# Attention, its first pair of heads, and the transfers around it: one change to a fused attention and two-layer-expert kernel

## The chip, the core and the metric

The kernel runs on one core of a Trainium2 chip. A core has five engines that run side by side and wait for one another through semaphores: TensorE (PE, matrix products and transposes), VectorE (DVE), ScalarE (ACT), GpSimd (POOL) and SyncE (SP), which here only issues transfers. Transfers are carried by 16 DMA engines that all the issuing engines share. SBUF is the memory on the core (128 partitions), PSUM holds what TensorE writes (8 banks of 128 x 512 float32), HBM is the memory outside. The metric is the time of one execution on the device in microseconds (us); of several runs the median counts.

## The reference, cut to what matters

```python
# attention: batch 2, 8 heads, 768 rows, head size 64; 16 heads in all
q_bits = (q @ proj > 0); k_bits = (k @ proj > 0)          # 6 bits each
mask   = bucket(q_bits)[:, None] == bucket(k_bits)[None, :]
scores = where(mask, q @ k.T / 8, -1e9)
attn   = softmax(scores); attn_out = attn @ v
# first expert layer (dense), 1536 tokens x 512, inner size 2048
h = x @ w_in;  g = (a0 + a1 h + a2 h^2 + a3 h^3) / (1 + |b0||h| + |b1| h^2 + 1e-6);  x = g @ w_out
# second layer: each token goes to its best of 8 experts
e = argmax(x @ w_gate);  out = prob[e] * (relu(x @ w1[e]) @ w2[e])
```

Products are made in float32 precision by splitting each operand into a high part and a low part (`hi`, `lo`).

## The kernel before, in words

The program has three stages: attention (to about 306 us of the profile), the dense layer (to about 600 us) and the routed experts.

**Attention** works on heads in pairs, 8 pairs. PE's work is written out by hand in slots, 24 to a pair, 201 in all: even slots make a block of scores (L1195, L1196), three slots in four make a chunk of four transposes of exponentials (L1205), and from slot 9 on each slot makes one value product, `pv` (L1217, L1218), which sums into bank 6. A head's output is finished in two halves of six value products; ACT then copies bank 6 out (`o_evict`, L747), and the next `pv` waits for that copy (`o_out`, L1214). ACT makes the exponentials (L730) and the high parts (L739), DVE the maxima (L940) and the low parts (L960).

The next pair is prepared in the slots of the present one, in ten steps (`step`) that share bank 7: four transposes of q and k, copied to `raw` (L717, L928); POOL splits them into `qk_hi` and `qk_lo` (L571, L573); products with `proj` give `bits` (L720), and two products with `sel` give `mask` (L931, L934). The first pair goes through the same ten steps before slot 0. `raw` and `qk_lo` are the same memory, so ACT's copy for pair p waits until the operands of both heads of pair p-1 have landed (L716).

**SP's queue** is one list, in order: the operands of the two heads of a pair (five transfers each, L453 to L457, waiting for the split), their masks (L464), the loads of q and k (L439) and of v (L444), the output rows (L480, L481), the inverse sums, which go out to HBM (`inverse`, L469) and come back spread over partitions (`rb`, L473), and `routed<-blank` (L514): 21 writes of 128 rows of 2,056 bytes that clear the buffer for the routed tokens. After the last pair SP loads the second quarter of the dense layer's weights (L524, L525), which ACT splits from its step n = 6 on (`w_piece(1, 0)`, L762); ACT works in order, so everything behind that split waits for the load.

Of the kernel before, what the change touches and what calls it, by code (L numbers as in the profile page):

```python
# [15 lines left out]
P = 128  # L16
# [34 lines left out]
C_END = C_TILE + NTAB  # L51


def constants():

    c = np.zeros((P, C_END), np.float32)
# [24 lines left out]
def build(nc, q, k, v, proj, w_in, w_out, a, b, w_gate, w1, w2, consts, out):  # L81
    ctx = ExitStack()
    with ctx:
# [63 lines left out]
        vn = [put(f"vn{i}", [P, NT * D], F32) for i in range(2)]  # L147
        vs = [put(f"vs{i}", [P, NT, 2 * D], F32R) for i in range(2)]
        blank = put("blank", [P, ROW], F32)
        bits = put("bits", [P, HALF], BF16)  # L150
# [78 lines left out]
        s_blank = sem("s_blank")  # L229
# [11 lines left out]
        v_split = sem("v_split")  # L241
        prep_pe = sem("prep_pe")
# [102 lines left out]
        TURN_R_AT = 5  # L345
# [23 lines left out]
        def prep_no(p, k):  # L369

            return 10 * p + k if p < 2 else 20 + 11 * (p - 2) + k + (k >= 4)

        def turn_r_no(p):

            return 20 + 11 * p + 4 if p < NPAIR - 2 else 20 + 11 * (NPAIR - 2) + p - (NPAIR - 2)
# [54 lines left out]
        def _(sp):  # L430
            sp.dma_start(cst[:, 0:P], consts[:, 0:P]).then_inc(s_ident, 16)

            def load_qk(p):

                if p >= 2:
                    sp.wait_ge(prep_pe, prep_no(p - 2, 3) + 1)
# [4 lines left out]
            def load_v(n):  # L441

                wait(sp, v_split, 2 * (n - 1))
                sp.dma_start(vn[n % 2][:, :], v_h[n, :, :]).then_inc(s_v[n % 2], 16)  # L444

            def operand_rows(p):

                sp.wait_ge(qk_split, 4 * (p + 1))
                wait(sp, scores_ready, 12 * (p - 1))
                for o in range(2):  # L450
                    own, other = slice(o * D, (o + 1) * D), slice((1 - o) * D, (2 - o) * D)
                    op, landed = operands[p % 2][o], s_op[p % 2][o]
                    sp.dma_start(op[own, 0:2, :].bitcast(F32), qk_hi[own, 0:1, :].bitcast(F32).broadcast_to([D, 2, S])).then_inc(landed, 16)  # L453
                    sp.dma_start(op[other, 0, :].bitcast(F32), qk_lo[own, 0, :].bitcast(F32)).then_inc(landed, 16)
                    sp.dma_start(op[own, 2, :].bitcast(F32), qk_hi[own, 1, :].bitcast(F32)).then_inc(landed, 16)
                    sp.dma_start(op[other, 2, :].bitcast(F32), qk_hi[own, 1, :].bitcast(F32)).then_inc(landed, 16)
                    sp.dma_start(op[own, 3, :].bitcast(F32), qk_lo[own, 1, :].bitcast(F32)).then_inc(landed, 16)  # L457

            def mask_rows(p):

                sp.wait_ge(prep_out, prep_no(p, 9) + 1)
                for o in range(2):
                    own, other = slice(o * D, (o + 1) * D), slice((1 - o) * D, (2 - o) * D)
                    sp.dma_start(operands[p % 2][o][other, 1:4:2, :].bitcast(F32), mask[own, 0:2, :].bitcast(F32)).then_inc(s_op[p % 2][o], 16)  # L464

            def inverse_rows(p):

                sp.wait_ge(prep_out, turn_r_no(p) + 1)
                sp.dma_start(inverse[p, :, :].rearrange("h (t c) -> (h t) c", c=P), rt[0:2 * NT, :]).then_inc(s_inverse, 16)  # L469
                sp.wait_ge(s_inverse, 16 * (p + 1))  # L470
                wait(sp, x_norm, p)
                for o in range(2):
                    sp.dma_start(rb[o * D:(o + 1) * D, :], inverse[p, o:o + 1, :].broadcast_to([D, S])).then_inc(s_rb, 16)  # L473
# [9 lines left out]
            load_qk(0)  # L483
            sp.dma_start(cst[:, P:C_END], consts[:, P:C_END]).then_inc(s_const, 16)
            sp.dma_start(pr_raw[0:D, :], proj).then_inc(s_proj, 16)
            sp.dma_start(pr_raw[D:P, :], proj).then_inc(s_proj, 16)
            load_qk(1)
            load_v(0)
            load_v(1)
# [918 lines left out]
```

## Time and profile before

| what | us |
|---|---|
| median of 3 runs (lowest, highest) | 931.68 (929.39, 936.72) |
| the profiled execution, its own time | 933.58 |
| its span, first to last instruction | 931.8 |
| attention, first block of scores to the last value product | 33.0 to 305.3 |
| PE busy in the span | 805.1 (86%) |
| mean granted TensorE clock | 0.954 of full speed |

The profile gives for each engine what it did and when, and for each idle time what ended it. A time in a row is counted from the start of the span. A matrix product's own row has its duration as modelled; where PE is idle over a stretch this is seen from the idle time before a row. For transfers a row of SPq is the issue, and the time to landing is given apart.

### The profile page before, as it was taken

To read this page: it belongs to the slowest core of one execution; us is meant where nothing else is said; L and a number is where in the kernel's file an instruction comes from. 1 tells how busy PE (TensorE), PEld (TensorE's weight loads), DVE (VectorE), ACT (ScalarE), POOL (GpSimd) and SP (SyncE) were. 2 spreads that over 40 slices of the span, in tenths; PEclk is the share of its full clock that TensorE was granted. 3 is DMA by queue.
4 is the path that set the end of the run, shared out by engine and by line. 5 is a ranking of instruction groups with operands and counts; after the bars stand their busy time and mean duration, and the time that the engine had idled before them with its cause. 6 is when DMAs were issued, how large, how long until landed. Compare 5 with 4: busy or idle time off the path is not lost.

```text
span 931.8 us, 14695 instructions
## 1 busy us (share of the span) xinstructions
PE 805.1 (86%) x4212; PEld 701.0 (75%) x4212; DVE 666.7 (72%) x1068; ACT 641.4 (69%) x1248; POOL 457.3 (49%) x373
## 2 busy tenths in 40 slices
PE   3599999989988989999999997914999999898984
PEld 2488888878878879999999996903777777686763
DVE  1388787777776678787887886172788886895863
ACT  2377677767778887788787765233888887784871
POOL 3213552453347587476575543054357656553453
PEclk9999999999999999999999998856999999899898
DMA  5797688678671302002000300028531014115550
GB/s 140 153 226 190 155 200 213 164 168 212 142 219 37 124 1 64 28 1 91 1 1 1 152 30 1 1 102 329 189 126 45 30 38 183 59 45 200 217 192 16
DMA packets 59444, 104.52 MB, mean 112 GB/s; under 512 B 30622, under 2 KB 32894, under 8 KB 55296
## 3 DMA queue, kind: packets, MB, share of 16 engines
q1 hardware_dynamic: 53888, 92.04, 34.4%
q10 hardware_dynamic: 3024, 5.53, 2.1%
q0 software_dynamic: 2480, 6.31, 1.8%
q8 instruction: 26, 0.43, 0.2%
q14 instruction: 26, 0.21, 0.1%
HBM read 60.52 MB, written 13.71 MB: 80 GB/s over the span
## 4 chain that ended last, share of the span: by engine, by line
PE 52%; DMA 11%; issue 11%; SPq 7%; ACT 6%; DVE 5%; POOL 5%; ACTq 2%; DVEq 1%; POOLq 0%
PE ps L1252 4%; PE ps L1251 4%; PE ps L1253 4%; PE ps L1267 4%; PE ps L1269 4%; PE ps L1268 4%; DMA out<-yo,gi 4%; DMA operand<-mask 4%; PE ps L1205 4%; PE ps L1369 3%; PE ps L1370 3%; PE ps L1371 3%; PE ps L1195 2%; PE ps L1217 2%; PE ps L1196 2%
## 5 line engine op out<-in xcount | busy, mean ns | idle before, releaser
L960 DVE TENSOR_TENSOR ptl<-ps,pth 128x512 fp32r<-128x512 f32 x144 | 99.7, 692 | 46.6 <-ACT pth L739 43.7
L739 ACT ACTIVATE pth<-ps 128x512 fp32r<-128x512 f32 x144 | 86.1, 598 | 53.3 <-PE ps L1205 52.5
L856 ACT ACTIVATE e1h<-wraw 128x512 fp32r (+1 forms) x160 | 88.0, 619 | 34.2 <-DMA wraw<-in_moe_w 16.4
L940 DVE TENSOR_REDUCE negmax<-ps 128x1 f32<-128x768 f32 x96 | 91.4, 952 | 23.1 <-PE ps L1196 21.7
L631 POOL TENSOR_TENSOR hw<-hw,ha 128x384 f32<-128x384 f32 x64 | 65.6, 1025 | 83.2 <-ACT hw L803 83.2
L856 ACT ACTIVATE e2h<-wraw 128x512 fp32r (+1 forms) x152 | 86.2, 624 | 14.9 <-PE ps L1371 13.0
L730 ACT ACTIVATE pr<-ps,negmax 128x768 f32<-128x768 f32 x96 | 86.5, 901 | 14.1 <-DVE negmax L940 14.1
L1123 DVE TENSOR_TENSOR e1l<-wraw,e1h 128x512 fp32r<-128x512 f32 x120 | 78.8, 719 | 17.5 <-ACT e1h L856 17.3
L1205 PE MATMUL ps<-cst,pr 128*128 128x128 f32 x576 | 89.2, 276 | 1.2 <-ACT pr L730 1.2
L676 POOL TENSOR_TENSOR e2l<-wraw,e2h 128x512 fp32r<-128x512 f32 x38 | 51.3, 1353 | 79.0 <-DVE e2l L1123 53.6
L1251 PE MATMUL ps<-xh,wih 128*128 128x384 f32 x256 | 87.5, 342 | 2.0 <-DVE hp L996 2.0
L1123 DVE TENSOR_TENSOR e2l<-wraw,e2h 128x512 fp32r<-128x512 f32 x114 | 85.7, 817 | 4.1 <-issue 2.7
L1217 PE MATMUL ps<-pth,vs 128*128 128x384 f32 x192 | 77.9, 405 | 12.3 <-issue 6.0
L1252 PE MATMUL ps<-xl,wih 128*128 128x384 f32 x256 | 87.0, 340 | 0.0
L1253 PE MATMUL ps<-xh,wil 128*128 128x384 f32 x256 | 87.0, 340 | 0.0
L1195 PE MATMUL ps<-operand 128*128 128x384 f32 x192 | 70.8, 369 | 13.3 <-DMA operand<-mask 13.3
L1369 PE MATMUL ps<-e2h,hth 128*128 128x512 f32 x152 | 64.6, 425 | 18.4 <-DVE htl L1110 18.4
L426 POOL TENSOR_TENSOR gl<-ha,gh 128x384 fp32r<-128x384 f32 x64 | 65.4, 1022 | 27.9 <-ACT gh L420 27.8
L1267 PE MATMUL ps<-woh,gh 128*128 128x512 f32 x192 | 76.0, 396 | 3.0 <-POOL gl L426 3.0
L1205 PEld LDWEIGHTS ps<-cst,pr 128*128 128x128 f32 x576 | 72.2, 142 | 7.9 <-ACT pr L730 2.3
L1269 PE MATMUL ps<-woh,gl 128*128 128x512 f32 x192 | 75.5, 393 | 0.0
L1268 PE MATMUL ps<-wol,gh 128*128 128x512 f32 x192 | 75.5, 393 | 0.0
(170 smaller groups left out, 2221.1 us busy)
## 6 DMA issues: line engine op xcount, KB each, us to landing
wraw<-in_moe_w SPq DMA_DIRECT2D x32, 1024.0 KB, 8.7
operand<-qk_hi SPq DMA_DIRECT2D x16, 384.0 KB, 4.9
operand<-qk_lo SPq DMA_DIRECT2D x32, 192.0 KB, 4.3
operand<-qk_hi SPq DMA_DIRECT2D x32, 192.0 KB, 4.5
operand<-mask SPq DMA_DIRECT2D x16, 384.0 KB, 6.3
routed<-blank SPq DMA_DIRECT2D x21, 257.0 KB, 4.8
xg<-routed ACTq DMA_DIRECT2D x21, 257.0 KB, 2.7
wi_raw<-in_moe_w_in SPq DMA_DIRECT2D x4, 1024.0 KB, 6.1
```

The lines of the kernel that those rows point to most:

```text
L856: act.activation(E_HI[x][:, k, :], raw_piece(at, x, k), ACT.Copy).then_inc(e_hi[x], 1)
L960: dve.tensor_tensor(ptl[:, at:at + CW], ps[:, 4 + c % 2, :], pth[:, at:at + CW].bitcast(F32), ALU.subtract).then_inc(ptl_done, 1)
L1123: dve.tensor_tensor(E_LO[x][:, k, :], raw_piece(at, x, k), E_HI[x][:, k, :].bitcast(F32), ALU.subtract).then_inc(e_lo_dve[x], 1)
L1205: mm = pe.transpose(ps[:, 4 + c % 2, x * P:(x + 1) * P], pr[u % UNITS][:, t, kt * P:(kt + 1) * P], ident)
L1217: pe.matmul(ps[:, 6, 0:HALF], vs[n % 2][:, kt, :], pth[:, cols], start=(kt == 0), stop=False)
L1251: pe.matmul(bank, wh[:, kt, f], xh[:, bb * KD + kt, cols], start=(kt == 0), stop=False)
L1252: pe.matmul(bank, wh[:, kt, f], xl[:, bb * KD + kt, cols], start=False, stop=False)
L1253: mm = pe.matmul(bank, wl[:, kt, f], xh[:, bb * KD + kt, cols], start=False, stop=(kt == KD - 1))
L1267: pe.matmul(ps[:, 4 + t, :], gh[s % 2][:, m, rows], woh[qq % 2][:, m, :], start=(m == 0), stop=False)
L1268: pe.matmul(ps[:, 4 + t, :], gh[s % 2][:, m, rows], wol[qq % 2][:, m, :], start=False, stop=False)
L1269: mm = pe.matmul(ps[:, 4 + t, :], gl[s % 2][:, m, rows], woh[qq % 2][:, m, :], start=False, stop=(m == M4 - 1))
L1369: pe.matmul(ps[:, 2 + par, :], hth[par][:, kt, :], e2h[:, kt, :], start=(kt == 0), stop=False)
```

## The change

- **First pair.** Q loads are issued by SP, k loads by ACT. The four groups of transposes go to banks 0 to 3 without waiting for one another; the second half is split by ACT and DVE instead of POOL; the products of bits and masks have banks of their own (4 to 7, 0, 1). On SP the first head's five operands and its mask go ahead of the second head's.
- **Value product.** The first `pv` of each half head is issued one slot later, behind that slot's scores and ahead of its transposes. The transpose of the inverse sums goes from slot 5 to slot 6 of a pair.
- **Transfers.** V comes for two heads at once. `rb` comes back in one transfer of 2 x 64 rows instead of two of 64. In SP's list the first head's operands stand between `inverse` out and `rb` in.
- **Clearing.** The 21 writes from SBUF are taken out of the pairs. After the last output rows and ahead of the weights there are 7 transfers from HBM to HBM, each of 3 x 128 rows, read from a block appended to the constants and repeated three times.

```diff
@@ order of the value product and of the inverse's transpose @@
-        TURN_R_AT = 5
+        TURN_R_AT = 6
...
+                j = s - FIRST_PV
+                if j > 0 and (j - 1) % NT == 0:
+                    pv(j - 1)
                 for c in chunks_at(s):
                     turn(c)
-                if s >= FIRST_PV:
-                    pv(s - FIRST_PV)
+                if j >= 0 and j % NT:
+                    pv(j)
@@ SP @@
-                for o in range(2):
-                    sp.dma_start(rb[o * D:(o + 1) * D, :], inverse[p, o:o + 1, :].broadcast_to([D, S])).then_inc(s_rb, 16)
+                sp.dma_start(rb[:, :], inverse[p, :, :].unsqueeze(1).broadcast_to([2, D, S])).then_inc(s_rb, 16)
...
+                sp.dma_start(vn[p % 2][:, :, :], v_h[2 * p:2 * p + 2, :, :].rearrange("o p x -> p o x")).then_inc(s_v[p % 2], 16)
...
+                if p >= 1:
+                    inverse_out(p - 1)
                 if p + 1 < NPAIR:
-                    load_v(2 * p + 2)
+                    operand_rows(p + 1, 0)
                 if p >= 1:
-                    inverse_rows(p - 1)
+                    inverse_in(p - 1)
                 if p + 1 < NPAIR:
-                    operand_rows(p + 1)
+                    operand_rows(p + 1, 1)
                 if p >= 1:
                     o_rows(2 * p - 1)
                 if p + 1 < NPAIR:
-                    load_v(2 * p + 3)
-                for t in range(3 * p, min(3 * p + 3, NROUTED)):
-                    sp.dma_start(routed[t * P:(t + 1) * P, :], blank[:, :]).then_inc(s_blank_out, 16)
-                if p + 1 < NPAIR:
-                    mask_rows(p + 1)
+                    load_v(p + 1)
+                    mask_rows(p + 1, 0)
+                    mask_rows(p + 1, 1)
                 o_rows(2 * p)
...
             o_rows(NHEAD - 1)
+            for t in range(0, NROUTED, 3):
+                sp.dma_start(routed[t * P:(t + 3) * P, :].rearrange("(t p) r -> t p r", p=P),
+                             consts[:, C_BLANK:C_BLANK + ROW].unsqueeze(0).broadcast_to([3, P, ROW])).then_inc(s_blank_out, 16)
             for n in range(1, NQ):
@@ ACT, first pair @@
+            for o in range(2):
+                act.dma_start(nat[0][:, 1, :, o, :], k_h[o, :, :, :]).then_inc(s_qk[0], 16)
+            for half in range(2):
+                act.wait_ge(first_pe, 2 * half + 1)
+                act.activation(raw[:, 0, half * HALF:(half + 1) * HALF], ps[:, 2 * half, 0:HALF], ACT.Copy, scale=0.125).then_inc(first_act, 1)
...
+            act.wait_ge(first_dve, 2)
+            act.wait_ge(first_act, 2)
+            act.activation(qk_hi[:, :, HALF:S], raw[:, :, HALF:S], ACT.Copy).then_inc(first_hi, 1)
@@ DVE, first pair @@
+            dve.wait_ge(first_hi, 1)
+            dve.tensor_tensor(qk_lo[:, :, HALF:S], raw[:, :, HALF:S], qk_hi[:, :, HALF:S].bitcast(F32), ALU.subtract).then_inc(first_lo, 1)
```

SP's list in one pair before, from the inverse sums to the first mask (`operand_70` and `operand_88` are the two heads of the next pair, `osb_75` the output of a head that is done):

```order
L469 DMA inverse<-rt 12x128 [waits prep_out]
L473 DMA rb<-inverse 64x768 [waits s_inverse]
L473 DMA rb<-inverse 64x768
L453 DMA operand_70<-qk_hi 64x2x768 [waits scores_ready,qk_split]
...
L453 DMA operand_88<-qk_hi 64x2x768
...
L480 DMA o_hi<-osb_75 64x768 [waits o_out]
L481 DMA o_lo<-osb_75 64x768
L444 DMA vn_79<-in_v 128x384 [waits v_split]
L514 DMA routed<-blank 128x514 x3
L464 DMA operand_70<-mask 64x2x768 [waits prep_out]
```

and of the change:

```order
L481 DMA inverse<-rt 12x128 [waits prep_out]
L463 DMA operand_70<-qk_hi 64x2x768 [waits scores_ready,qk_split]
...
L487 DMA rb<-inverse 128x1x768 [waits s_inverse]
L463 DMA operand_87<-qk_hi 64x2x768 [waits scores_ready,qk_split]
...
L494 DMA o_hi<-osb_75 64x768 [waits o_out]
L495 DMA o_lo<-osb_75 64x768
L451 DMA vn_78<-in_v 128x2x384 [waits v_split]
L476 DMA operand_70<-mask 64x2x768 [waits prep_out]
```

The clearing is gone from between v and the mask, one load of v is gone, and `rb` stands between the two heads' operands.

SP's list at the end of attention before:

```order
L469 DMA inverse<-rt 12x128 [waits prep_out]
L473 DMA rb<-inverse 64x768 [waits x_norm,s_inverse]
L473 DMA rb<-inverse 64x768
L480 DMA o_hi<-osb_75 64x768 [waits x_lo,o_out]
L481 DMA o_lo<-osb_75 64x768
L524 DMA wi_raw<-in_moe_w_in 128x4x512 [waits w_lo,w_hi]
L525 DMA wo_raw<-in_moe_w_out 128x4x512
```

and of the change:

```order
L481 DMA inverse<-rt 12x128 [waits prep_out]
L487 DMA rb<-inverse 128x1x768 [waits x_norm,s_inverse]
L494 DMA o_hi<-osb_75 64x768 [waits x_lo,o_out]
L495 DMA o_lo<-osb_75 64x768
L536 DMA routed<-in_consts 384x1x514 x7
L542 DMA wi_raw<-in_moe_w_in 128x4x512 [waits w_lo,w_hi]
L543 DMA wo_raw<-in_moe_w_out 128x4x512
```

The seven clearing transfers stand ahead of the weights' second quarter.

## Rows read from the trace of the kernel before

**Rows 1.** The page: the span, and the busiest engine.
```profile
span 931.8 us, 14695 instructions
PE 805.1 (86%) x4212; PEld 701.0 (75%) x4212; DVE 666.7 (72%) x1068; ACT 641.4 (69%) x1248; POOL 457.3 (49%) x373
```

**Rows 2.** Stages: us, busy of PE, PEld, DVE, ACT, POOL, clock, DMA share, GB/s.
```profile
80.00:130.00 50.00, 45.93 (x294) 41.22 (x293) 39.58 (x58) 37.67 (x77) 20.18 (x16) 1.00 0.84 203
180.00:230.00 50.00, 45.69 (x284) 41.20 (x283) 37.97 (x57) 36.19 (x74) 17.52 (x14) 0.97 0.82 197
```

**Rows 3.** Waits of PE, 33 to 306 us: total, times, longest.
```profile
PE ps L1195 <- DMA operand<-mask: 13.3, 6, 8.1
PE ps L1217 <- issue: 6.0, 8, 3.7
PE ps L1217 <- POOL vs L583: 4.0, 6, 0.7
PE ps L1184 <- DVE raw L928: 2.4, 6, 0.4
PE ps L1217 <- ACT osb L747: 1.3, 1, 1.3
```

**Rows 4.** Timeline before and at slot 0: start, us, engine, line.
```profile
3.36 0.65 SPq L439 DMA_DIRECT2D nat<-in_k  x1
7.47 0.87 PE L1164 MATMUL ps<-cst,nat 128*128 128x128 f32 x3 [7.47 <-DMA nat<-in_k]
...
15.88 1.81 POOL L573 TENSOR_TENSOR qk_lo<-raw,qk_hi 128x768 fp32r<-128x768 f32 x1
...
17.72 0.67 SPq L453 DMA_DIRECT2D operand<-qk_hi  x1
...
27.99 1.87 SPq L464 DMA_DIRECT2D operand<-mask  x2
...
32.99 0.69 PE L1195 MATMUL ps<-operand 128*128 128x384 f32 x1 [8.13 <-DMA operand<-mask]
...
36.63 0.48 ACT L717 ACTIVATE raw<-ps 128x384 f32<-128x384 f32 x1
```

**Rows 5.** Timeline of one pair's operands, 105 to 130 us.
```profile
105.42 1.83 POOL L573 TENSOR_TENSOR qk_lo<-raw,qk_hi 128x768 fp32r<-128x768 f32 x1
108.86 0.64 SPq L453 DMA_DIRECT2D operand<-qk_hi  x1
...
121.60 1.60 SPq L514 DMA_DIRECT2D routed<-blank  x3
123.25 1.36 SPq L464 DMA_DIRECT2D operand<-mask  x2
...
129.19 0.44 PE L1195 MATMUL ps<-operand 128*128 128x384 f32 x1 [1.05 <-DMA operand<-mask]
```

**Rows 6.** DMA packets, 105.6 to 107.5 us, one inverse<-rt and nothing else.
```profile
DMA packets 24, 0.01 MB, mean 3 GB/s; under 512 B 12, under 2 KB 24, under 8 KB 24
```

**Rows 7.** DMA packets, 108.8 to 120 us: operands, with ten completions.
```profile
DMA packets 968, 2.49 MB, mean 222 GB/s; under 512 B 160, under 2 KB 160, under 8 KB 967
```

**Rows 8.** DMA packets, 89.5 to 91.5 us: mostly the clearing's rows.
```profile
DMA packets 380, 0.68 MB, mean 342 GB/s; under 512 B 41, under 2 KB 82, under 8 KB 379
```

**Rows 9.** DMA packets, 311.5 to 315.5 us: the weights' second quarter.
```profile
DMA packets 751, 1.51 MB, mean 376 GB/s; under 512 B 16, under 2 KB 16, under 8 KB 751
```

**Rows 10.** The page: the clearing's issues, KB each, us to landing.
```profile
routed<-blank SPq DMA_DIRECT2D x21, 257.0 KB, 4.8
```

**Rows 11.** Timeline of SP's last transfers of attention, and the weights' first.
```profile
306.01 1.10 SPq L473 DMA_DIRECT2D rb<-inverse  x2
307.21 0.54 SPq L480 DMA_DIRECT2D o_hi<-osb  x1
307.80 0.60 SPq L481 DMA_DIRECT2D o_lo<-osb  x1
308.49 0.54 SPq L524 DMA_DIRECT2D wi_raw<-in_moe_w_in  x1
309.07 0.58 SPq L525 DMA_DIRECT2D wo_raw<-in_moe_w_out  x1
```

**Rows 12.** DMA issues, 304.7 to 330 us: KB each, us to landing.
```profile
wo_raw<-in_moe_w_out SPq DMA_DIRECT2D x1, 1024.0 KB, 9.4
```

**Rows 13.** Timeline of ACT: its first split of the second quarter.
```profile
330.61 0.61 ACT L762 ACTIVATE wih<-wi_raw 128x512 fp32r<-128x512 f32 x1
```

More of the change, by code:

```diff
@@ L459, in mask_rows, with load_v @@
[L459 to L466, printed above, removed]
+            def load_v(p):
+                wait(sp, v_split, 4 * (p - 1))
+                sp.dma_start(vn[p % 2][:, :, :], v_h[2 * p:2 * p + 2, :, :].rearrange("o p x -> p o x")).then_inc(s_v[p % 2], 16)
@@ new lines, in operand_rows @@
+            def operand_rows(p, o):
+                if p:
+                    sp.wait_ge(qk_split, 4 * p + 2)
+                else:
+                    sp.wait_ge(qk_split, 2)
+                    sp.wait_ge(first_lo, 1)
+                wait(sp, scores_ready, 12 * (p - 1))
+                own, other = slice(o * D, (o + 1) * D), slice((1 - o) * D, (2 - o) * D)
+                op, landed = operands[p % 2][o], s_op[p % 2][o]
+                sp.dma_start(op[own, 0:2, :].bitcast(F32), qk_hi[own, 0:1, :].bitcast(F32).broadcast_to([D, 2, S])).then_inc(landed, 16)
+                sp.dma_start(op[other, 0, :].bitcast(F32), qk_lo[own, 0, :].bitcast(F32)).then_inc(landed, 16)
+                sp.dma_start(op[own, 2, :].bitcast(F32), qk_hi[own, 1, :].bitcast(F32)).then_inc(landed, 16)
+                sp.dma_start(op[other, 2, :].bitcast(F32), qk_hi[own, 1, :].bitcast(F32)).then_inc(landed, 16)
+                sp.dma_start(op[own, 3, :].bitcast(F32), qk_lo[own, 1, :].bitcast(F32)).then_inc(landed, 16)
@@ L468, in inverse_rows, with mask_rows, inverse_out @@
+            def mask_rows(p, o):
+                if p:
+                    sp.wait_ge(prep_out, prep_no(p, 9) + 1)
+                else:
+                    sp.wait_ge(first_dve, 6)
+                own, other = slice(o * D, (o + 1) * D), slice((1 - o) * D, (2 - o) * D)
+                sp.dma_start(operands[p % 2][o][other, 1:4:2, :].bitcast(F32), mask[own, 0:2, :].bitcast(F32)).then_inc(s_op[p % 2][o], 16)
+            def inverse_out(p):
                 sp.wait_ge(prep_out, turn_r_no(p) + 1)
@@ L591, in norm_x @@
             def norm_x(p):
[L593 removed]
+                pool.wait_ge(s_rb, 16 * (p + 1))
                 pool.wait_ge(x_sum, p + 1)
@@ L704, in _ @@
                 act.activation(wproj[rows, x // 2 * 2, x * NBITS:(x + 1) * NBITS], pr_raw[rows, :], ACT.Copy).then_inc(proj_hi, 1)
+            act.wait_ge(first_dve, 2)
+            act.wait_ge(first_act, 2)
+            act.activation(qk_hi[:, :, HALF:S], raw[:, :, HALF:S], ACT.Copy).then_inc(first_hi, 1)
+            act.wait_ge(s_const, 16)
+            act.activation(sel[:, :], cst[:, C_SEL:C_SEL + 2 * P], ACT.Copy).then_inc(sel_made, 1)
+            for half in range(2):
+                act.wait_ge(first_pe, 5 + half)
+                act.activation(bits[:, half, :], ps[:, 4 + half, 0:HALF], ACT.Sign, bias=cst[:, C_TINY:C_TINY + 1]).then_inc(first_act, 1)
             def step(p, k):
@@ L719, in step @@
                     act.wait_ge(prep_pe, m + 1)
-                    act.activation(bits[:, :], bank, ACT.Sign, bias=cst[:, C_TINY:C_TINY + 1]).then_inc(prep_out, 1)
+                    act.activation(bits[:, half, :], bank, ACT.Sign, bias=cst[:, C_TINY:C_TINY + 1]).then_inc(prep_out, 1)
             def exps(g):
@@ L762, in w_piece @@
                 act.activation(dst[:, p_ % 4, :], src[:, p_ % 4, :], ACT.Copy).then_inc(w_hi, 1)
-            for k in range(10):
-                step(0, k)
             act.wait_ge(s_coef, 32)
@@ L911, in _ @@
             dve.memset(coef[:, 10:11], 1.0 + 1e-6).then_inc(coef_made, 1)
+            for half in range(2):
+                dve.wait_ge(first_pe, 2 * half + 2)
+                dve.tensor_copy(raw[:, 1, half * HALF:(half + 1) * HALF], ps[:, 2 * half + 1, 0:HALF]).then_inc(first_dve, 1)
             dve.wait_ge(proj_hi, 4)
@@ L1176, in step @@
                     pe.wait_ge(sel_made, 1)
-                    mm = pe.matmul(bank, sel[:, x * P:(x + 1) * P], bits[:, :], start=True, stop=True)
+                    mm = pe.matmul(bank, sel[:, x * P:(x + 1) * P], bits[:, half, :], start=True, stop=True)
                 mm.then_inc(prep_pe, 1)
```

110 lines of the change are left out of this document (65 added, 45 removed).

## The prediction, made before the result was known

> **What bounds the kernel now.** I read the page first: the span is 931.8 us and PE is busy for 805.1 of it [rows 1]. Then the stages by windows: in attention PE works 45.9 of 50 us at a full clock, DVE 39.6 and ACT 37.7, and the DMA engines are 84% busy at 203 GB/s [rows 2]. So PE is the bound there, with some 4 us in 50 to gain, and the transfers are close behind it. Then PE's waits, by what ended them [rows 3]: 13.3 us for the masks of a pair, of which 8.1 is the first pair and 5.2 five later ones; 11.3 us at the first value product of a half head (6.0, 4.0 and 1.3; the sixth to eleventh product is never waited for, and POOL's split is long done where it is named: what they wait for is ACT's copy of bank 6); 2.4 us at the transpose of the inverse sums. Last the timelines of the places that the change touches: the beginning [rows 4], one pair's operands [rows 5], the end of attention [rows 11, 13].
>
> The sum is made against the profiled execution's 933.6 us; the median of the runs is 1.9 below it, which I take off at the end.
>
> **First pair.** SP issues four loads one by one, the last at 3.36, and PE starts at 7.47 [rows 4]. With two of them issued by ACT the last goes out some 0.7 to 1.3 us earlier; the four carry 0.79 MB, which at 222 GB/s [rows 7] takes 3.5 us from about 3.0: PE starts at about 6.5. The four groups of transposes (0.87 us one after the other, less when they overlap) end 2.8 us later. POOL's split of the first half ends at 6.5 + 2.1 (two transposes and DVE's copy) + 0.8 + 1.8 = 11.3. ACT and DVE make the second half's from about 10.2 in 0.9 and 1.0 us: 12.1. The operands' first transfer goes out at 12.1 instead of 17.72 [rows 4], 5.6 us earlier. Before, ten transfers took SP 10.3 us (17.72 to 27.99) and the first mask landed 5 us after its issue, 32.99 [rows 4]. Now the first head needs five and a mask: 12.1 + 4.9 = 17.0; the mask (four products with `sel`, four DVE passes) is ready near 17.8; first scores near 22, 11 us earlier. But that isn't what counts: `raw` shares memory with `qk_lo`, so ACT's first copy for the next pair waits for the second head's mask too. This goes out at 18.6 + 5.1 = 23.7 and lands 5 us later, 28.7. The copy stood at 36.63 [rows 4]. I take **-7.9 us**; the ends are -5.6 (only the earlier start stays) and -10.9 (the copy isn't waited for).
>
> **Value product and inverse, on PE.** Moved a slot later, the product finds bank 6 copied; scores fill the place. Of 11.3 us I count 7 as gained where PE alone sets the pace: 0.33 and some 0.4 of 0.66 in each pair (the `sel` product that comes forward then waits for ACT's `bits`), and 2.3 in the last pair, where ACT is held by its weights. The transpose in slot 6 finds its bank free: 2.4 gained. POOL, ACT and DVE do nothing more or less for it. This is only worth something while PE sets the pace, which the transfers decide.
>
> **Transfers inside a pair.** Before, 20.3 us pass from the first operand's issue at 108.86 to the scores at 129.19 [rows 5]. In them lie rb 0.39 MB, ten operands 2.36, rows 0.39, v 0.20, clearing 0.79, first mask 0.39: 4.5 MB, or 222 GB/s, what [rows 7] has. The stretch is bound by transfers. Now the operands go at 107.3, when POOL's split ends [rows 5], and clearing is gone.
>
> What decides is how many of the 16 DMA engines a transfer uses. The trace has one transfer whose row count is no multiple of 16: the 12 rows of `inverse`. Its 24 packets are 12 of data and 12 small ones that report completion [rows 6]; ten transfers on 16 engines have 160 small ones [rows 7]. So twelve rows use twelve engines: the outer count is what is dealt out. Two transfers of the change have sides with different outer counts: `rb` reads 2 x 64 rows into 128, the clearing reads 3 x 128 into 384. No row shows such a one. The ends are all 16 engines, and 2 and 3 of them. I take 2 and 3, since in [rows 6] nothing was cut finer to fill the other engines.
>
> The Trainium skill ("DMA: Bandwidth & Descriptors", in the section on why a DMA increments its semaphore by 16) says so outright: the number is the largest up to 16 that divides both sides' slowest dimension. By it these would run on 2 and 3 engines. For 12 rows the trace agrees; for unlike sides no row shows it.
>
> Each engine works off its list in order. Per engine, at 222 to 376 GB/s over 16 [rows 7, 9], `rb` on two engines is 0.197 MB: 8.4 to 14.2 us, against 1.8 before. On those two engines the mask lies behind the first head's operands (5.3 us at 222), `rb` (9.2 at the 342 of [rows 8]) and 2.36 MB more, which takes 6.3 to 10.6, say 8.4, as the other fourteen run dry: 22.9 us, scores at 130.2, or **+1 us per pair** for the six pairs that have an `rb` before their mask: +6. The ends: all at 222, 107.3 + 15.9 + 14.2 = 137.4, +8.2 a pair, +49; all at 376, mask not waited for and PE's moves paid, -2.5 a pair, -15. PE's own gains then stay only in the first and last pair: **-2.5**.
>
> **Clearing.** Taken from the pairs it frees 0.79 MB each, counted above. Placed ahead of the weights it is 21 x 257 KB = 5.5 MB [rows 10]. On three engines that is 1.84 MB each: 78 us at 376, 86 at 342 [rows 8, 9]. Two of the three have `rb` ahead, until about 306.0 + 1.5 + 9.2 = 316.7 [rows 11]; the clearing ends at 395 to 403, and the weights' share behind it (2.1 MB at 376, 5.6 us) lands at 401 to 408. ACT needs them at 330.61 [rows 13] and works in order; behind its split stand the reading of PE's banks, DVE's polynomial, POOL's low parts and so PE, which has two banks in hand. Only ACT's wait shows: 70 to 78 us, **+74**. PE comes back at the low clock for a few us, as after the 3.7 us wait in the last pair: +1.7. The cover before was that the load had landed at 318.5 [rows 11, 12], 12.1 us early. The removed memsets on POOL ran before anything needed POOL: nothing.
>
> **Sum.** 933.6 - 7.9 - 2.5 + 6 + 74 + 1.7 = 1004.9, less 1.9: **1003 us**. Its own range adds the ends: 973 (-10.9, -15, +70) to 1055 (-5.6, +49, +78).
>
> **Rivals.**
> A, the other side: all 16 engines carry both transfers. Point of decision: `rb` lands within about 4 us and the mask after the first operand in under 20 us. Then the stretch is 3.9 MB, 17.7 us at 222: scores could start at 125, before PE is there. PE's pace rules: -7 - 2.4 - 4.6 of the later masks' 5.2, -1.5 for the low clock that follows the longest of them (0.97 in [rows 2]); clearing takes 14.7 to 16.2 us against 12.1 to spare: +3.5. 933.6 - 7.9 - 15.5 + 3.5 - 1.9 = 912 us (903 to 922). For it: transfers of this trace are dealt evenly whenever they can be, and the rows to move are 128 and 384. Against it: [rows 6].
> B: `rb` is narrow but the clearing is dealt evenly over its 128 rows: 933.6 - 7.9 - 2.5 + 6 + 3.5 - 1.9 = 931 us. For it: nothing but that the two are of unlike shape.
> C: three engines, and HBM to HBM costs a packet its read and its write one after the other: another 78 us, 1082. Against it: reading rows and writing rows each move at 342 to 376, and an engine overlaps them in both.
>
> **How the numbers follow.** The forecast 66%, A 22%, B 6%, C 6%. The predicted time is the forecast's, 1003. Its own range is 973 to 1055; the range given, 910 to 1045, takes in nearly all of it (63%), B and over half of A: 81%. 1% of the time, about what a measurement can tell, is 9.3 us, so faster is below 922: A but for its upper end, 20%. Within 1%: B and the rest of A, 7%. Slower: 73%.
>
> **What would show it.** Right: ACT's first `wih` of the second quarter waits 70 us or more for a transfer of weights, PE is idle with it, and the DMA share there is near 3 in 16 at some 65 to 75 GB/s; `rb` takes over 10 us to land, and PE waits for a mask in pairs 2 to 7. First pair: ACT's copy of `raw` near 28.7. Value product: no wait of L1251 over 0.3 us but in the last pair. Wrong: DMA share near 1 in the clearing and `rb` landing in 4 us; then A stands. Were ACT's wait far from 74 us with three engines at work, the price per packet was wrong, not the mechanism.

## The result, and the profile after

The changed kernel takes 1050.77 us (median of 4 runs, 1046.96 to 1056.94); the kernel before, run beside it, 932.73. The ratio is 1.127, with a 95% interval of 1.120 to 1.134. Ratios here and below compare fast executions alone, so they can differ a little from the ratio of the two medians. The forecast was 1003 with a range to 1045: the sign and both mechanisms were right, the size of one term was not. The profiled execution took 1056.94 us, its span 1055.2.

The page, the line of the span and that of the busiest engines, against [rows 1]:

```profile
span 1055.2 us, 14664 instructions
PE 822.6 (78%) x4212; PEld 720.0 (68%) x4212; DVE 666.1 (63%) x1069; ACT 641.3 (61%) x1249; POOL 456.9 (43%) x369
```

DVE, ACT and POOL do what they did, within 1 us each. PE is busy 17.5 us longer with the same 4212 products: it ran longer at the low clock (mean granted clock 0.886 instead of 0.954). The rest of the 123 us by which the span is longer is idle time of PE. Two stretches of attention by windows (columns as in [rows 2]), and one behind it:

```profile
80.00:130.00 50.00, 38.90 (x236) 35.64 (x235) 31.34 (x48) 29.98 (x61) 14.58 (x12) 0.86 0.64 139
180.00:230.00 50.00, 33.02 (x197) 30.30 (x197) 26.07 (x39) 24.71 (x50) 16.54 (x14) 0.83 0.52 116
400.00:430.00 30.00, 0.00 (x0) 0.00 (x0) 0.00 (x0) 0.00 (x0) 0.00 (x0) 0.51 0.20 71
```

In attention PE lost 7 to 13 us of 50, and the DMA engines, 84% busy before, are at 64 and 52%. A resource that got idler together with PE can be a sign that a few of its parts carry the load. Between 400 and 430 us no engine works at all, at a DMA share of 0.20 and 71 GB/s.

PE's waits between 33 and 310 us, the costliest first, against [rows 3]:

```profile
PE ps L1229 <- DMA operand<-mask: 45.5, 5, 9.5
PE ps L1198 <- ACT raw L747: 7.1, 4, 6.5
PE ps L1211 <- DVE mask L968: 3.9, 13, 0.3
PE ps L1198 <- DVE raw L965: 2.5, 7, 0.7
```

Five masks are waited for 9.1 us each, and a sixth, at 315.35, for 9.12. The waits at the first value product and at the inverse's transpose (13.7 us before) are gone from the list. One pair, first SP's queue and then the block of scores that waits, against [rows 5]:

```profile
115.55 0.65 SPq L463 DMA_DIRECT2D operand<-qk_hi  x1
...
120.43 0.74 SPq L487 DMA_DIRECT2D rb<-inverse  x1
...
129.18 1.41 SPq L476 DMA_DIRECT2D operand<-mask  x2
```
```profile
144.09 0.69 PE L1229 MATMUL ps<-operand 128*128 128x384 f32 x1 [8.90 <-DMA operand<-mask]
```

From the first operand's issue to the scores 28.5 us pass instead of 20.3. The packets say why, first from 118 to 134 us, then from 137 to 143:

```profile
DMA packets 1390, 3.34 MB, mean 209 GB/s; under 512 B 192, under 2 KB 416, under 8 KB 1389
```
```profile
DMA packets 115, 0.26 MB, mean 43 GB/s; under 512 B 16, under 2 KB 48, under 8 KB 115
```

209 GB/s over 16 engines is 13 GB/s for one. From 137 us on two of the 16 are left with work (two of 16 are a share of 0.125; in windows of 1 us the share is 0.12 to 0.14), at 43 GB/s, 21.5 each. The scores that wait for the mask start at 144.09, when these two are about done.

The end of attention: ACT's first split of the second quarter of the weights, against [rows 13], and the clearing's packets from 388 to 438 us:

```profile
454.73 0.63 ACT L791 ACTIVATE wih<-wi_raw 128x512 fp32r<-128x512 f32 x1 [70.25 <-DMA wo_raw<-in_moe_w_out]
```
```profile
DMA packets 1736, 3.54 MB, mean 71 GB/s; under 512 B 14, under 2 KB 14, under 8 KB 1736
```

Where the 123 us went, by these marks: the last value product ends at 358.5 instead of 305.2, +53.3; ACT then waits 70.25 us for the weights, and its first split comes 124.1 us later than at 330.61 [rows 13]. Everything behind it takes as long as before. The prediction had +74 for the clearing, and a wait of 70.25 came; for everything in attention it had -4.4, and attention ended 53.3 later.

### The profile page after: what moved, and what is told of

It reads as the page before. It is cut to its first block, busy times and chain, and to the rows that moved or that the text cites. A ratio compares the mean times of both kernels' runs of the same rounds, so it can differ in the third digit from the quotient of the medians.

```text
span 1055.2 us, 14664 instructions
## 1 busy us (share of the span) xinstructions
PE 822.6 (78%) x4212; PEld 720.0 (68%) x4212; DVE 666.1 (63%) x1069; ACT 641.3 (61%) x1249; POOL 456.9 (43%) x369
## 4 chain that ended last, share of the span: by engine, by line
PE 38%; DMA 17%; SPq 16%; issue 10%; DVE 6%; ACT 5%; POOL 4%; ACTq 2%; DVEq 1%; POOLq 0%
DMA operand<-mask 8%; SPq L536 6%; DMA out<-yo,gi 5%; PE ps L1312 3%; PE ps L1311 3%; PE ps L1313 3%; PE ps L1327 3%; PE ps L1328 3%; PE ps L1329 3%; PE ps L1239 3%; PE ps L1429 2%; DVE e2l L1157 2%; PE ps L1431 2%; PE ps L1430 2%; SPq L465 2%
## 5 line engine op out<-in xcount | busy, mean ns | idle before, releaser
L1229 PE MATMUL ps<-operand 128*128 128x384 f32 x192 | 76.1, 396 | 59.9 <-DMA operand<-mask 59.9
L1028 DVE TENSOR_TENSOR hp<-ps,hp 128x384 f32<-128x384 f32 x64 | 35.5, 554 | 94.0 <-ACT hp L827 93.8
L1239 PE MATMUL ps<-cst,pr 128*128 128x128 f32 x576 | 94.2, 287 | 0.6 <-ACT pr L760 0.5
L1311 PEld LDWEIGHTS ps<-xh,wih 128*128 128x128 f32 x256 | 49.0, 191 | 66.6 <-DVE hp L1030 65.0
L609 POOL TENSOR_TENSOR o_hi<-o_hi,o_lo 128x768 f32<-128x768 f32 x8 | 14.5, 1809 | 163.1 <-DMA o_lo<-osb 163.1
L1229 PEld LDWEIGHTS ps<-operand 128*128 128x128 f32 x192 | 40.0, 208 | 62.6 <-DMA operand<-mask 62.5
L1239 PEld LDWEIGHTS ps<-cst,pr 128*128 128x128 f32 x576 | 75.9, 149 | 8.8 <-ACT pr L760 1.7
```

The source lines that it names most:

```text
L1229: pe.matmul(bank, operand_of(n, 0)[:, rows], operand_of(n, 2)[:, cols], start=True, stop=False)
L1239: mm = pe.transpose(ps[:, 4 + c % 2, x * P:(x + 1) * P], pr[u % UNITS][:, t, kt * P:(kt + 1) * P], ident)
L1311: pe.matmul(bank, wh[:, kt, f], xh[:, bb * KD + kt, cols], start=(kt == 0), stop=False)
```

## The experiments

Twelve kernels, each timed against the kernel before on the same chip; medians of the kernel before lay between 933.2 and 934.1. The theory: a transfer whose two sides have different outer counts runs on few DMA engines, 2 for `rb` and 3 for the clearing, and what stands behind it on those waits. The rival: SP's new order, the later value product, or copies from HBM to HBM as such.

### Each narrow transfer made wide, alone and together

`rb` in two transfers (label rb_two):

```diff
-                sp.dma_start(rb[:, :], inverse[p, :, :].unsqueeze(1).broadcast_to([2, D, S])).then_inc(s_rb, 16)
+                for o in range(2):
+                    sp.dma_start(rb[o * D:(o + 1) * D, :], inverse[p, o:o + 1, :].broadcast_to([D, S])).then_inc(s_rb, 16)
```

> The changed kernel, with `rb` brought back in two transfers of 64 rows, as before the change. Theory 1 (narrow transfers: `rb` runs on 2 of 16 engines, and everything behind it on those two waits): the five waits of PE for a mask between 33 and 310 us, 45.5 us together, fall below 8, the spacing of the pairs from 43 to about 33.3 us, `rb` lands in under 4 us; six pairs x 9.6 = 58 us come back: 993 us (985 to 998). The wait of ACT for the weights stays near 70. Theory 2 (the new place of `rb` between the two heads' operands, or the order of SP's list as such, holds the masks up): the waits stay at 9 us each, 1045 to 1055 us.

Measured: 992.5 us, ratio 1.062 [1.059, 1.066]; 58.3 us came back, where 58 were expected. Some 6 of them lie behind the pairs: ACT's wait for the weights is 64.3 us instead of 70.2, since the last narrow `rb` stood ahead of the clearing on two of its three engines. PE's waits for masks up to 360 us, the first pair's 5.3 among them:

```profile
PE ps L1230 <- DMA operand<-mask: 17.3, 7, 5.3
```

They didn't fall below 8, as both the theory and rival A of the prediction had it: some 12 us are left in six pairs. That is followed up below.

The clearing as 128 x 3 rows on both sides (clear_wide):

```diff
-                sp.dma_start(routed[t * P:(t + 3) * P, :].rearrange("(t p) r -> t p r", p=P),
-                             consts[:, C_BLANK:C_BLANK + ROW].unsqueeze(0).broadcast_to([3, P, ROW])).then_inc(s_blank_out, 16)
+                sp.dma_start(routed[t * P:(t + 3) * P, :].rearrange("(t p) r -> p t r", p=P),
+                             consts[:, C_BLANK:C_BLANK + ROW].unsqueeze(1).broadcast_to([P, 3, ROW])).then_inc(s_blank_out, 16)
```

> The changed kernel, with the same seven clearing transfers written as 128 x 3 rows on both sides instead of 3 x 128 against 384. Theory 1 (three engines): 128 rows are dealt over 16 engines, the clearing takes 5.5 MB at 340 to 380 GB/s = 14.5 to 16 us instead of 78, ACT's wait for the weights falls from 70.2 to 5 to 9 us: 1050.8 - 63 = 988 us (983 to 993). Theory 2 (HBM to HBM is slow as such, whatever the number of engines): the rate stays near 71 GB/s or at least under 150, the wait stays over 25 us, the time over 1005.

Measured: 991.0 us, ratio 1.061 [1.059, 1.064]. The same seven transfers of the same bytes from HBM to HBM; only which count stands outermost has changed. The DMA engines from 362 to 377 us:

```profile
362.00:377.00 15.00, 12.82 (x65) 10.83 (x63) 12.26 (x22) 13.97 (x29) 10.72 (x10) 1.00 1.07 268
```

The rate is 268 GB/s instead of 71, and ACT's wait 11.7 us instead of 70.2. I had expected a wait of 5 to 9, from a rate of 340 to 380. Theory 2 is out.

Both edits (both_wide):

> The changed kernel with both transfers over 16 engines (`rb` in two transfers of 64 rows, clearing as 128 x 3 rows). Theory 1: both gains add, 1050.8 - 58 - 63 = 930, less what PE gains by the change's other parts once masks are not waited for, 5 to 12 us: 918 to 930 us, so narrow transfers are the whole of the loss. Theory 2 (another part of the change loses time as well, for instance the order of SP's list or the later value product): over 936.

Measured: 937.9 us, ratio 1.005 [1.002, 1.008]. The gains add nearly in full (112.9 of 118.1 us; the last `rb`, which stood ahead of the clearing, is counted in both), so the narrow transfers are practically the whole loss. But the change still isn't faster than the kernel before, where rival A had 912: something else eats what it was to bring.

### Is it the outer count, and is it a queue?

The clearing as three transfers of 7 x 128 rows (clear_seven):

```diff
-            for t in range(0, NROUTED, 3):
-                sp.dma_start(routed[t * P:(t + 3) * P, :].rearrange("(t p) r -> t p r", p=P),
-                             consts[:, C_BLANK:C_BLANK + ROW].unsqueeze(0).broadcast_to([3, P, ROW])).then_inc(s_blank_out, 16)
+            for t in range(0, NROUTED, 7):
+                sp.dma_start(routed[t * P:(t + 7) * P, :].rearrange("(t p) r -> t p r", p=P),
+                             consts[:, C_BLANK:C_BLANK + ROW].unsqueeze(0).broadcast_to([7, P, ROW])).then_inc(s_blank_out, 16)
```

> The changed kernel with the clearing as three transfers of 7 x 128 rows instead of seven of 3 x 128. Theory 1 (the outer count is the number of engines, 7 here, and each moves 23.7 GB/s as in the changed kernel, 71 / 3): 5.5 MB at 166 GB/s take 33 us instead of 78, ACT's wait for the weights falls from 70 to 26 us: 1050.8 - 45 = 1006 us (1000 to 1012), DMA share 0.44 instead of 0.20. Theory 2 (the number of rows in an instruction or HBM to HBM as such sets the rate): 1040 to 1055.

Measured: 1008.1 us, ratio 1.079 [1.075, 1.084]; the wait is 26.4 us. The windows show the seven engines, at a share of 0.46 and 23 GB/s for each:

```profile
380.00:385.00 5.00, 1.47 (x7) 1.34 (x8) 3.23 (x7) 2.62 (x5) 5.00 (x5) 1.00 0.46 162
...
390.00:395.00 5.00, 4.16 (x21) 3.35 (x19) 0.00 (x0) 0.00 (x0) 0.00 (x0) 1.00 0.46 164
```

3, 7 and 16 engines: 71, 163 and 268 GB/s. The Trainium skill ("DMA: Bandwidth & Descriptors", in the section on why a DMA increments its semaphore by 16) gives as the number of engines the largest one up to 16 that divides the slowest dimension of both sides. The rows agree: 3 engines for 3 and 384, 7 for 7 and 896, 16 for 128 and 128.

Half of `rb`'s columns narrow, half wide (rb_half):

```diff
-                sp.dma_start(rb[:, :], inverse[p, :, :].unsqueeze(1).broadcast_to([2, D, S])).then_inc(s_rb, 16)
+                sp.dma_start(rb[:, 0:HALF], inverse[p, :, 0:HALF].unsqueeze(1).broadcast_to([2, D, HALF])).then_inc(s_rb, 16)
+                for o in range(2):
+                    sp.dma_start(rb[o * D:(o + 1) * D, HALF:S], inverse[p, o:o + 1, HALF:S].broadcast_to([D, HALF])).then_inc(s_rb, 16)
```

> The changed kernel with half the columns of `rb` brought in by the one narrow transfer (2 engines) and the other half by two transfers of 64 rows (16 engines). Theory 1 (the price is the queue of the two engines, bytes over their rate): an engine of the two carries 98 + 12 KB of it instead of 197, where evenly dealt it is 25; the excess falls from 172 to 86 KB and the 58.3 us that the run with two transfers gave back fall to half, 1050.8 - 29 = 1022 us (1015 to 1028), the mask waits from 9.1 to about 5 us. Theory 2 (a fixed price of a narrow transfer, whatever its bytes): 1045 to 1050.

Measured: 1025.5 us, ratio 1.098 [1.092, 1.103]. PE's waits for masks from 33 to 360 us:

```profile
PE ps L1231 <- DMA operand<-mask: 31.3, 6, 6.0
```

5.2 us each instead of 9.1, and 25.2 of the 58.3 us came back: the price goes with the bytes that the two engines carry, so it is a queue and no fixed price of such a transfer.

The narrow `rb` behind the masks (rb_behind):

```diff
-                if p >= 1:
-                    inverse_in(p - 1)
                 if p + 1 < NPAIR:
                     operand_rows(p + 1, 1)
...
                     mask_rows(p + 1, 1)
+                if p >= 1:
+                    inverse_in(p - 1)
                 o_rows(2 * p)
```

> The changed kernel with the narrow `rb` issued behind both masks of the pair instead of between the two heads' operands. Theory 1 (not `rb` itself but what stands behind it on its two engines is late): the mask waits of 9 us go. `rb` then lands some 12 us after the mask's issue and POOL, which normalizes before it splits the next q and k, is late: 12 + 5.5 (normalizing) + 6 (two splits) + 13.6 (operands to mask in SP's queue) = 37 us from pair to pair instead of 42.9: 1050.8 - 6 x 5.9 = 1015 us (1005 to 1025), the wait turned into one for POOL. Theory 2 (the narrow transfer costs wherever it stands): 1045 to 1055.

Measured: 1036.2 us, ratio 1.107 [1.101, 1.113], 11 us over the upper end of what theory 1 gave. POOL's waits from 90 to 310 us, and PE's from 33 to 360:

```profile
POOL o_hi L615 <- DMA rb<-inverse: 63.7, 6, 11.4
```
```profile
PE ps L1202 <- POOL qk_lo L593: 25.1, 5, 5.6
PE ps L1251 <- issue: 14.3, 1, 14.3
PE ps L1229 <- DMA operand<-mask: 8.2, 5, 2.5
```

The masks' waits fall to 8.2 us, nearly as expected, and the wait turned into one for POOL: 39.6 us from pair to pair, where I had 37. POOL starts the product with `rb` at 139.97, 13.7 us after SP issued it at 126.30, so `rb` takes that long to land. Another 14 us are in the last pair, where `rb` stands ahead of the weights' first quarter in SP's list: the weights go out 13.9 us after that pair's first scores (305.79 - 291.92) instead of 6.2 in the changed kernel, ACT waits 13.7 us for them, PE 14.3. So in the one place the masks behind `rb` pay for the two slow engines, in the other POOL, which needs `rb` itself, and the weights. Neither theory's range holds the 1036.2.

### The clearing behind the weights

```diff
@@ behind the issue of the second quarter's weights @@
+                if n == 1:
+                    for t in range(0, NROUTED, 3):
+                        sp.dma_start(routed[t * P:(t + 3) * P, :].rearrange("(t p) r -> t p r", p=P),
+                                     consts[:, C_BLANK:C_BLANK + ROW].unsqueeze(0).broadcast_to([3, P, ROW])).then_inc(s_blank_out, 16)
```

> The changed kernel with the clearing as it is (3 engines), but issued behind the second quarter's weights instead of ahead of them. Theory 1 (the weights stand behind 1.84 MB on three of their engines; only the order makes it cost): the clearing still takes about 78 us at some 71 GB/s, ACT's wait of 70.2 us falls below 1, nobody waits for the clearing: 1050.8 - 72 = 979 us (974 to 984). Theory 2 (the memory or the engines are kept so busy by HBM to HBM copies that other loads are slowed too): the weights still land late or later loads are waited for, over 990.

Measured: 993.5 us, ratio 1.065 [1.062, 1.068]: 57 of the 72 us came back. Nobody waits for the second quarter. SP's queue shows a new delay:

```profile
359.09 1.23 SPq L540 DMA_DIRECT2D wo_raw<-in_moe_w_out  x1
360.37 73.84 SPq L543 DMA_DIRECT2D routed<-in_consts  x7
434.31 10.93 SPq L539 DMA_DIRECT2D wi_raw<-in_moe_w_in  x1
445.29 1.09 SPq L540 DMA_DIRECT2D wo_raw<-in_moe_w_out  x1
```

These narrow transfers hold not only their engines but the issuing queue: SP is 73.8 us in issuing seven, and the third quarter goes out from 434 to 446 us. ACT waits 8.4 us for it. The two theories are both partly right. In the profiled execution the experts' stage begins 63.9 us earlier than in the changed kernel (690.76 against 754.62), which with the 8.4 makes the 72. The medians give 57, and what makes the difference isn't settled: the four executions of this run lie between 988 and 998, and the profiled one is the fastest of them.

### What is left: wide transfers, and where the gain went

Both wide and the clearing behind the weights (best):

> Both transfers over 16 engines, and the clearing issued behind the second quarter's weights. Theory 1 (what is left of the clearing's price in the run with both wide is ACT's wait of 9.7 us for the weights, 341.77 against 330.61): that wait goes, 937.9 - 9.7 = 928 us (925 to 931), no gain or a gain of half a per cent over the kernel before. Theory 2 (the clearing costs elsewhere too, by the memory it keeps busy, or by the third quarter of the weights coming late): 933 or more.

Measured: 936.2 us, ratio 1.006 [1.002, 1.011]: theory 1 fell. ACT's first split comes at 329.54 instead of 341.77, so its wait is gone, and yet the experts' stage begins only 3.4 us earlier (635.43 against 638.78). ACT's wait had mostly been covered by what PE had in hand: PE waits 3.2 us for `hp`, DVE's polynomial of the dense layer, in both_wide, and 2.0 in best. PE waits for masks in this kernel as in rb_two:

```profile
PE ps L1231 <- DMA operand<-mask: 12.6, 6, 2.7
```

The same with the old order of the value product (pv_old):

```diff
-        TURN_R_AT = 6
+        TURN_R_AT = 5
...
-                if j > 0 and (j - 1) % NT == 0:
-                    pv(j - 1)
...
-                if j >= 0 and j % NT:
+                if j >= 0:
                     pv(j)
```

> As the run called best, with the order on PE as before the change: the first value product of a half head in its old slot, the inverse's transpose in slot 5. Theory 1 (the later product takes 5 us or so of waiting out of PE's path, as the prediction of rival A has it): 928 + 5 = 933 us. Theory 2 (the transfers of a pair set the pace; what PE saves it waits for the mask): 927 to 929, with mask waits shorter by what the old waits cost. Theory 3 (the longer mask waits drop the granted clock, so the later product loses): under 925.

Measured: 932.5 us, ratio 1.004 [0.999, 1.008]; its waits from 33 to 310 us:

```profile
PE ps L1253 <- issue: 8.1, 9, 5.5
PE ps L1200 <- ACT raw L749: 7.6, 7, 6.3
PE ps L1253 <- POOL vs L605: 4.0, 6, 0.7
PE ps L1231 <- DMA operand<-mask: 3.9, 5, 1.0
```

The old waits are back (8.1 and 4.0) and the mask's fell by 8.7: time is mostly moved between them. The 932.5 meets theory 1's 933 by luck: its base of 928 for best was never reached. Against best as measured, the later product loses 3.7 us in the medians and 3.5 at the start of the experts' stage, the sign of theory 3. The two intervals against the kernel before overlap, but the two runs were made on one chip, twelve executions each, and compared directly their means are 3.1 us apart, with a 95% interval of about 0.8 to 5.4. The cause is argued and not tried by itself: the clock, from 180 to 230 us in best and then in pv_old:

```profile
180.00:230.00 50.00, 45.05 (x283) 40.80 (x281) 38.03 (x57) 36.19 (x75) 17.43 (x14) 0.97 0.76 175
```
```profile
180.00:230.00 50.00, 45.66 (x293) 40.87 (x292) 40.02 (x58) 37.68 (x78) 22.05 (x18) 1.00 0.73 164
```

How it is lost is clearest in both_wide, at 94 to 98 us, behind a wait of 1.8 us for a mask, and at 104 to 108:

```profile
94.00:98.00 4.00, 4.00 (x20) 3.77 (x21) 2.32 (x3) 1.90 (x4) 3.78 (x5) 0.65 0.00 1
104.00:108.00 4.00, 4.00 (x27) 3.87 (x27) 3.73 (x7) 3.24 (x7) 3.03 (x3) 1.00 0.03 6
```

This wait costs more than itself: behind it the granted clock is 0.65 of full speed, some of the time at its lower level of 1.2 GHz, and 20 products are made in 4 us instead of 27. The length of a wait alone doesn't decide it: a wait of 1.69 us at 128.56 in the same run left the clock at 1.00, and of best's six waits for a mask (1.4 to 2.7 us) two were followed by 0.50. In pv_old five waits of 0.2 to 0.7 us between 102 and 130 us, 1.9 in all, left it at 1.00.

The load of v for both heads moved out of the busy stretch (v_early):

```diff
                     load_qk(p + 2)
+                if p + 1 < NPAIR:
+                    load_v(p + 1)
...
-                    load_v(p + 1)
                     mask_rows(p + 1, 0)
```

> As best, with the load of v for both heads of a pair issued behind that of q and k, while the DMA engines are nearly idle, instead of ahead of the masks. Theory 1 (a pair is bound by the bytes between its first operand and its mask, 3.9 MB in 19 us; masks are waited for 1.3 to 2.1 us in four of six pairs and the clock falls behind such waits): 0.39 MB less, 1.9 us a pair, waits near 0, 928 - 8 = 920 us (916 to 924), PE's clock in attention 0.99 or more instead of 0.97. Theory 2 (the mask is late for another reason, when DVE makes it or SP comes to it): 926 to 929 us.

Measured: 923.8 us, ratio 0.990 [0.984, 0.995]: the first that beats the kernel before, by 1%. The time is in theory 1's range, but the step from best is 12.4 us in the medians, where 8 had been expected from 928. The waits for masks fall to 1.5 us in all. Windows from 80 to 130 and from 180 to 230 us:

```profile
80.00:130.00 50.00, 47.67 (x312) 43.22 (x311) 41.84 (x62) 39.90 (x82) 22.91 (x19) 1.00 0.73 165
180.00:230.00 50.00, 48.01 (x317) 44.01 (x316) 42.33 (x64) 39.28 (x81) 26.82 (x22) 1.00 0.70 157
```

PE is busy 1.7 to 2.3 us more in 50 than before [rows 2]. So part of the gain that rival A had counted, some 10 of its 20 us, was there, and 0.39 MB in the wrong place had taken it.

The first head's mask ahead of the second head's operands, and the coefficients' loads early, beside the edit of v_early (order):

```diff
             load_v(0)
+            sp.dma_start(coef[:, 0:4], a.rearrange("(o n) -> o n", o=1).broadcast_to([P, 4])).then_inc(s_coef, 16)
+            sp.dma_start(coef[:, 4:6], b.rearrange("(o n) -> o n", o=1).broadcast_to([P, 2])).then_inc(s_coef, 16)
...
                     inverse_in(p - 1)
-                if p + 1 < NPAIR:
-                    operand_rows(p + 1, 1)
-                if p >= 1:
                     o_rows(2 * p - 1)
                 if p + 1 < NPAIR:
                     mask_rows(p + 1, 0)
+                    operand_rows(p + 1, 1)
                     mask_rows(p + 1, 1)
```

> As v_early, with the first head's mask issued ahead of the second head's operands, and the two small loads of coefficients ahead of the first pair's operands instead of behind its masks. Theory 1 (what the next pair needs first should go out first; in the first pair ACT's copy of raw stood behind a wait for those coefficients): no mask is waited for, ACT's copy comes at 30 to 31 us instead of 33.2: 920 - 4 = 916 us (911 to 920). Theory 2 (the second head's operands then hold up ACT's copy of raw of the next pair, a new wait of 1 to 3 us a pair): 922 to 935 us.

Measured: 915.0 us, ratio 0.983 [0.974, 0.991], in theory 1's range, though the step from v_early is 8.8 us and not 4. The run has two edits, and none tries them apart. No mask is waited for behind the first pair's. SP's queue in one pair shows the order. SP is idle for 3.5 us ahead of the mask's issue, so the mask now goes out when it is made and not when its turn comes:

```profile
109.72 0.60 SPq L496 DMA_DIRECT2D o_lo<-osb  x1
113.84 0.62 SPq L476 DMA_DIRECT2D operand<-mask  x1
114.56 0.62 SPq L463 DMA_DIRECT2D operand<-qk_hi  x1
```

The same with the old order of the value product (order_pv_old):

> As the run called order, with the first value product in its old slot and the inverse's transpose in slot 5. Theory 1 (the later product pays once transfers do not set the pace: 31.5 us from pair to pair instead of 33.0 to 33.3): seven pairs x 1.0 to 1.5 us, 915 + 9 = 924 us (920 to 927). Theory 2 (it loses here as it did in the run called best, or does nothing): 911 to 917.

Measured: 924.0 us, ratio 0.989 [0.986, 0.992], 9.0 us slower than order; the experts' stage begins at 622.49 instead of 612.24. The two ran on different chips, but the kernel before took nearly the same on both (934.1 beside order, 933.4 here), and the slowest execution of order (917.1) is faster than the fastest of this run (921.0). Here the later product pays, as it didn't between best and pv_old. It is the same edit in both, and the transfers decide what it is worth.

## Why the prediction was wrong, point by point

**What bounds the kernel.** Right, and "the transfers are close behind" more so than I used it: with both transfers wide it is they, not PE, that set a pair's pace.

**First pair: -7.9 forecast, -3.7 measured** at the mark that I had named, ACT's copy of `raw` (32.98 against 36.63). The first scores came 9.6 us earlier (23.39), 11 had been forecast. Two things were off. SP's two loads of coefficients had gone behind the masks, and ACT waits for them ahead of its first exponentials:

```profile
ACT coef L794 <- DMA coef<-in_moe_b: 14.6, 1, 14.6
```

In order, where they go early, the copy comes at 31.66, and what it waits for is the second head's mask:

```profile
31.66 0.49 ACT L748 ACTIVATE raw<-ps 128x384 f32<-128x384 f32 x1 [3.91 <-DMA operand<-mask]
```

So the coefficients are 1.3 of the missing 4.3 us. The others are in SP's queue: the second head's mask goes out at 25.89 instead of 23.7, since the first operand goes out at 13.47 instead of 12.1, and SP takes 6.9 us from the first mask's issue (19.01) to the second's, where I had 5.1.

Beside this, clock is lost around the first scores. The windows from the start:

```profile
0.00:24.00 24.00, 9.09 (x30) 7.03 (x31) 6.66 (x15) 5.30 (x12) 4.72 (x9) 0.95 0.82 180
24.00:36.00 12.00, 4.80 (x18) 3.80 (x17) 2.47 (x3) 2.44 (x7) 0.85 (x2) 0.50 0.79 168
```

The kernel before had a granted clock of 1.00 from 24 to 36 us, in spite of its wait of 8.13 us there [rows 4]. Why the clock held in the one and fell in the other isn't shown.

**Value product and inverse: -2.5 forecast.** The reason given for so little, "only worth something while PE sets the pace, which the transfers decide", is what the four runs show: no gain (+3.7) where transfers set the pace, -9.0 where they don't. Rival A's 9.4 us is near the second, but not in the place that it named: at the last value product order is 5.6 us ahead of order_pv_old (285.53 against 291.12), and the rest comes in the dense layer, whose code is the same in both. Why isn't known.

**Transfers inside a pair: +6 forecast, 58.3 measured (rb_two), some 52 of it in the pairs and 6 in ACT's wait. This step failed**, and it accounts for the miss nearly alone: 1003 + 46 = 1049 against 1050.8. The mechanism was the right one: two engines, and what stood behind `rb` was late. The error was in "9.2 at the 342 of rows 8" and "6.3 to 10.6, say 8.4": I let the two engines work at 21 GB/s each while the other fourteen were busy too. The trace after has 13 GB/s for an engine as long as all have work (209 over 16), and 21.5 when two are left, with the same kinds of transfers. An engine with 0.197 MB of `rb` is at the shared rate for most of it. My upper end, "all at 222", gave 30.1 us from the first operand to the scores, 28.5 were measured; my choice gave 22.9. The end that I called an end was the likelier case, since the fast rates in the rows before came from stretches with other kinds of transfers, writes to HBM [rows 8] and loads of weights [rows 9]. The measured time lies inside the forecast's own range, 973 to 1055, and above the 1045 that I gave: the upper end was cut off. (The terms of that upper end, -5.6, -2.5, +49, +78 and +1.7, add up to 1052; the 1055 leaves out the -2.5.)

The second part of the miss is the clock. I charged it once, behind the clearing, with 1.7 us. In the changed kernel it is lost at each of the six mask waits of 8.8 to 9.5 us; the windows behind the one of 9.5 us and later in the pair:

```profile
100.00:106.00 6.00, 5.10 (x20) 4.81 (x21) 2.09 (x3) 1.67 (x3) 5.63 (x6) 0.50 0.02 7
110.00:114.00 4.00, 4.00 (x30) 3.83 (x29) 3.40 (x5) 2.43 (x5) 2.74 (x3) 1.00 0.56 102
```

PE is at half clock, 1.2 GHz, for six us. By my reading the transposes of the next q and k are late by it, and so is POOL's split: the operands go out 14.7 us after a pair's first scores (115.55 - 100.90) instead of 13.3 (108.86 - 95.60), where I had put them 1.6 us earlier. The loop feeds itself: what the wait costs is added to the start of the transfers that the next wait is for. Stretch (+8.2) and start (+1.4) make the 9.6 us of this pair.

**Clearing: +74 forecast; the wait is 70.25 us**, and the run with a wide clearing gives back 59.8 us and keeps a wait of 11.7. Three engines, 71 GB/s, no engine of the core at work: as forecast. That the copies go from HBM to HBM has no price of its own beyond these rates: rival C is out.

**Rival A**, 912 us, was measured with both_wide at 937.9, so the mechanism that I gave 22% to would not have come out at its number either. It let the stretch without clearing take 17.7 us; it takes 21.4 (107.19 to 128.56). The clearing that was taken out is 0.79 MB, but 0.20 MB of v came in, and 3.9 MB over 222 GB/s leaves out the 1.3 us from the first issue to the first packet and the landing of the last. Rival B is out: the clearing ran on three engines in the changed kernel, and on seven in clear_seven.

**What stays open.** The kernel order begins its experts' stage 24.2 us before the kernel before does (612.24 against 636.44) and ends 18.9 before it in the profiled executions. This stage took 295 to 301 us in the runs here, whatever was edited ahead of it; why isn't settled. The split of 9.6 us between queue and clock is read from one trace and wasn't tried by itself. No run takes the new first pair out, so what it is worth in the whole time is known only from its marks.

## What to carry to other kernels

Before a transfer is merged or reshaped, look at the outermost count of both its sides: here it decided how many of the 16 engines worked, and a transfer on two or three of them held up what stood behind it on its engines, and a long row of them the issuing queue too. Price such a transfer at the rate that an engine has in the same company of transfers, not at the best rate in the trace. An edit that gives PE time was worth nothing here as long as PE waited for a transfer at the end of each round; take bytes out of that stretch and put first what is needed first, and then the same edit pays.

## What the runs showed of the hardware that I had not expected

- An engine's rate goes with how many work and with what they carry. With operands and masks between SBUF places it was 21.5 GB/s for each of two and 13 for each of sixteen (209 GB/s). From HBM to HBM it was 23.7 for each of three, 23 for each of seven and 17 for each of sixteen (268). But sixteen had 23.5 each with the loads of weights (376) [rows 9].
- The issuing queue is held up too: seven transfers on 3 engines kept SP for 73.8 us (clear_behind), on 16 engines for 15.3 (best).
- A wait of PE for a mask can cost granted clock, and its length alone doesn't decide it. Each of the changed kernel's six waits of 8.8 to 9.5 us was followed by some 3 to 6 us at 0.50. In both_wide waits of 1.81, 1.97, 2.13 and 2.18 us were followed by 0.50 within the next 4 us, and waits of 1.69 and 1.29 were not; in best waits of 2.13 and 2.15 were not either.
